# Fusing two MLP layers on one core: high and low weight halves stored side by side, column by column

## The reference

```python
w = softmax(weight, axis=-1)                       # 8 heads x 7 taps
x = causal_conv(x, w)                              # (2, 4096, 192) -> 8192 rows of 192
h = x @ moe_w_in;   x = maximum(0.01 * h, h) @ moe_w_out
h = x @ moe2_w_in
g = where(h >= 1, h, where(h <= -1, 0, (h + 1) ** 2 / 4))
out = g @ moe2_w_out                               # (8192, 192)
```

## Time and profile before

| | us |
|---|---|
| median of the runs | 1129.92 (1129.71 to 1130.29) |
| the profiled execution, its own time | 1129.76 |
| its span, from first to last instruction | 1128.0 |
| PE busy | 1116.7 (99%) |
| PEld busy | 921.9 (82%) |
| DVE busy | 896.7 (79%) |
| ACT busy | 798.2 (71%) |
| POOL busy | 50.0 (4%) |

### The profile page before, as it was taken

The page is one execution under the profiler, slowest core; times in us unless marked ns, Lnnn a source line. Parts: engine busy times, 40 slices in busy tenths (PEclk is TensorE's granted clock), DMA queues, the critical chain, the costliest instruction groups (busy, mean ns, idle before and its releaser), DMA issues.

```text
span 1128.0 us, 25723 instructions
## 1 busy us (share of the span) xinstructions
PE 1116.7 (99%) x9754; PEld 921.9 (82%) x9754; DVE 896.7 (79%) x1511; ACT 798.2 (71%) x1472; POOL 50.0 (4%) x76
## 2 busy tenths in 40 slices
PE   7999999999999999999999999999999999999998
PEld 6788888888888888888888888888888888888886
DVE  7787887888777887788877888787787877888665
ACT  6778667586675867758577685866758667686785
POOL 5543000000000000000000000000000000000000
PEclk9999999999999999999999999999999999999999
DMA  6330010101001010010100101001010100100001
GB/s 143 98 81 2 11 20 1 30 2 23 7 1 31 1 30 1 1 30 1 29 1 6 25 1 29 1 12 19 1 29 1 24 8 1 29 1 15 1 1 28
DMA packets 114568, 21.98 MB, mean 19 GB/s; under 512 B 106256, under 2 KB 114448, under 8 KB 114448
## 3 DMA queue, kind: packets, MB, share of 16 engines
q1 hardware_dynamic: 111600, 19.61, 9.7%
q10 hardware_dynamic: 2848, 0.75, 0.4%
HBM read 14.05 MB, written 6.29 MB: 18 GB/s over the span
## 4 chain that ended last, share of the span: by engine, by line
PE 96%; DVE 2%; ACT 1%; DMA 1%; issue 0%; ACTq 0%
PE acc_main L521 9%; PE acc_main L525 9%; PE acc_main L523 9%; PE acc_edge L513 9%; PE acc_edge L515 9%; PE hidden L443 9%; PE hidden L441 9%; PE hidden L445 9%; PE hidden L450 9%; PE hidden L457 5%; PE hidden L429 1%; PE acc_edge L487 1%; PE acc_main L497 1%; PE acc_main L493 1%; PE acc_main L495 1%; PE hidden L423 1%
## 5 line engine op out<-in xcount | busy, mean ns | idle before, releaser
L694 ACT CAST g_hi<-g 128x512 fp32r<-128x512 f32 x510 | 299.2, 618 | 271.9 <-PE acc_main L525 202.2
L963 DVE TENSOR_TENSOR g_lo<-g,g_hi 128x512 fp32r<-128x512 f32 x510 | 334.7, 690 | 95.8 <-ACT g_hi L694 91.2
L957 DVE SCALAR_TENSOR_TENSOR g<-hidden,pre 128x512 f32<-128x512 f32 x256 | 176.6, 690 | 105.2 <-ACT pre L682 102.3
L429 PE MATMUL hidden<-op_edge,w_edge 64*128 64x512 f32 x768 | 255.7, 386 | 0.0
L423 PE MATMUL hidden<-op_hi,w_main 64*128 64x512 f32 x512 | 198.0, 387 | 3.3 <-DVE g L952 1.8
L441 PE MATMUL hidden<-op_hi,w_main 64*128 64x512 f32 x512 | 198.2, 387 | 0.0
L445 PE MATMUL hidden<-op_hi,w_main 64*128 64x512 f32 x512 | 197.9, 386 | 0.0
L425 PE MATMUL hidden<-op_lo,w_main 64*128 64x512 f32 x512 | 197.8, 386 | 0.0
L443 PE MATMUL hidden<-op_lo,w_main 64*128 64x512 f32 x512 | 197.7, 386 | 0.0
L450 PE MATMUL hidden<-op_edge,w_edge 64*128 64x512 f32 x512 | 197.7, 386 | 0.0
L427 PE MATMUL hidden<-op_hi,w_main 64*128 64x512 f32 x512 | 197.7, 386 | 0.0
(11 more groups left out here) (128 smaller groups left out, 2775.0 us busy)
## 6 DMA issues: line engine op xcount, KB each, us to landing
x_in<-in_x_dram SPq DMA_DIRECT2D x67, 64.0 KB, 2.2
out_dram<-y_main SPq DMA_DIRECT2D x62, 64.0 KB, 1.8
stage<-in_moe_w_out_dram SPq DMA_DIRECT2D x15, 192.0 KB, 2.7
x_in_edge<-in_x_dram SPq DMA_DIRECT2D x66, 32.0 KB, 2.0
out_dram<-y_edge SPq DMA_DIRECT2D x32, 64.0 KB, 1.8
stage<-in_moe_w_in_dram SPq DMA_DIRECT2D x15, 128.0 KB, 2.4
stage<-in_moe_w_in_dram SPq DMA_DIRECT2D x30, 64.0 KB, 2.4
stage<-in_moe_w_out_dram ACTq DMA_DIRECT2D x1, 192.0 KB, 4.5
```

Of the source, the lines that this page charges most:

```text
L429: done = nc.tensor.matmul(h[:], w_edge[l][top, i - 3, cols], op_edge[l][b][top, :], start=False, stop=False)
L694: nc.scalar.copy(hi_of(n, c)[:], g[c % SLOTS][:]).then_inc(g_hi_ready, 1)
L963: nc.vector.tensor_tensor(lo_of(n, c)[:], g[c % SLOTS][:], hi_of(n, c)[:].bitcast(F32), ALU.subtract).then_inc(g_lo_ready, 1)
```

## The change

Each weight's high and low part become neighbours. `w_main` and `w_edge` become [128, 2048, 2]; `w_out` becomes [128, 8, 3, 128, 2]: for a pair of chunks a block of main columns of the first chunk, one of the second (each column high, low), and a block of edge columns in which the innermost index is the chunk of the pair, with the high parts in columns 0 to 63 and the low ones in 64 to 127. A weight load still takes 128 columns, but steps 8 bytes from one to the next, over 1024 bytes of each partition. Sizes are unchanged, and so are all buffers' addresses. The number and order of matmuls, loads, DMAs and waits stay. Elementwise instructions that write weights now write (and POOL also reads) with an 8-byte step. ACT's third instruction of a piece becomes two, one of 256 columns and one of 128; in this last one, and in POOL's fourth, the staged input is read with the chunk as innermost index.

```diff
-        w_main = [sb(f"w_main{l}", [P, 2, F], F32R) for l in (0, 1)]
-        w_edge = [sb(f"w_edge{l}", [P, 2, F], F32R) for l in (0, 1)]
-        w_out = [sb(f"w_out{l}", [P, CHUNKS, 2 * D], F32R) for l in (0, 1)]
+        w_main = [sb(f"w_main{l}", [P, F, 2], F32R) for l in (0, 1)]
+        w_edge = [sb(f"w_edge{l}", [P, F, 2], F32R) for l in (0, 1)]
+        w_out = [sb(f"w_out{l}", [P, PAIRS, 3, P, 2], F32R) for l in (0, 1)]
...
-                nc.gpsimd.tensor_tensor(main[:, 1], s[:, 0:PW], main[:, 0].bitcast(F32), ALU.subtract)
+                nc.gpsimd.tensor_tensor(main[:, :, 1], s[:, 0:PW], main[:, :, 0].bitcast(F32), ALU.subtract)
...
-                nc.gpsimd.tensor_tensor(wo[:, :, 2 * P:], rows[:, :, 0:P], wo[:, :, 0:P].bitcast(F32), ALU.subtract)
-                nc.gpsimd.tensor_tensor(wo[:, :, D:2 * P], rows[:, :, P:D], wo[:, :, P:D].bitcast(F32),
-                                        ALU.subtract).then_inc(stage_used, 1)
+                nc.gpsimd.tensor_tensor(wo[:, 0:2, :, 1], rows[:, :, 0:P], wo[:, 0:2, :, 0].bitcast(F32), ALU.subtract)
+                nc.gpsimd.tensor_tensor(wo[:, 2, EDGE:P, :], rows[:, :, P:D].rearrange("p k c -> p c k"),
+                                        wo[:, 2, 0:EDGE, :].bitcast(F32), ALU.subtract).then_inc(stage_used, 1)
...
-                    nc.tensor.matmul(h[:], w_main[l][top, 0, cols], op_hi[l][b][top, :], start=True, stop=False)
+                    nc.tensor.matmul(h[:], w_main[l][top, cols, 0], op_hi[l][b][top, :], start=True, stop=False)
...
-                    nc.tensor.matmul(edge[:], w[:, P:2 * P], hi, start=k == 0, stop=False)
+                    nc.tensor.matmul(edge[:], w[:, 2, :, k % 2], hi, start=k == 0, stop=False)
...
-                    nc.tensor.matmul(main[:], w[:, 2 * P:], hi, start=False, stop=False)
+                    nc.tensor.matmul(main[:], w[:, k % 2, :, 1], hi, start=False, stop=False)
...
-                nc.scalar.copy(main[:, 0], s[:, 0:PW]).then_inc(weights_hi, 1)
-                nc.scalar.copy(edge[:, 0], s[:, PW:2 * PW]).then_inc(weights_hi, 1)
-                nc.scalar.copy(wo[:, :, 0:D], rows).then_inc(weights_hi, 1)
+                nc.scalar.copy(main[:, :, 0], s[:, 0:PW]).then_inc(weights_hi, 1)
+                nc.scalar.copy(edge[:, :, 0], s[:, PW:2 * PW]).then_inc(weights_hi, 1)
+                nc.scalar.copy(wo[:, 0:2, :, 0], rows[:, :, 0:P])
+                nc.scalar.copy(wo[:, 2, 0:EDGE, :], rows[:, :, P:D].rearrange("p k c -> p c k")).then_inc(weights_hi, 1)
```

More of the change, by code:

```diff
@@ L246, in piece_parts @@
             cols = slice(q * PW, (q + 1) * PW)
-            return (s, w_main[l][:, :, cols], w_edge[l][:, :, cols],
-                    s[:, 2 * PW:].rearrange("p (c d) -> p c d", d=D), w_out[l][:, q * PC:(q + 1) * PC])
+            return (s, w_main[l][:, cols, :], w_edge[l][:, cols, :],
+                    s[:, 2 * PW:].rearrange("p (c d) -> p c d", d=D), w_out[l][:, q])
         same = g[3][:, 0:P]
@@ L449, in bottom_first @@
                         pe.wait_ge(op1_ready, 1)
-                    done = nc.tensor.matmul(h[:], w_edge[l][bottom, 0, cols], op_edge[l][b][bottom, :],
+                    done = nc.tensor.matmul(h[:], w_edge[l][bottom, cols, 0], op_edge[l][b][bottom, :],
                                             start=False, stop=last)
@@ L456, in bottom_first @@
                         pe.wait_ge((op1_top_ready, op2_top_ready)[l], t + 1)
-                    nc.tensor.matmul(h[:], w_edge[l][bottom, 1, cols], op_top[l][b][bottom, :],
+                    nc.tensor.matmul(h[:], w_edge[l][bottom, cols, 1], op_top[l][b][bottom, :],
                                      start=False, stop=True).then_inc(hidden_ready, 1)
@@ L483, in top_second @@
                     pe.wait_ge(g_hi_ready, CHUNKS * n + k + 1)
[L484 removed]
+                    nc.tensor.matmul(edge[:], w[:, 2, :, k % 2], hi, start=k == 0, stop=False)
                 elif i in (1, 3):
                     pe.wait_ge(g_lo_ready, CHUNKS * n + k + 1)
[L487 removed]
+                    done = nc.tensor.matmul(edge[:], w[:, 2, :, k % 2], lo, start=False, stop=False)
                     if i == 3:
@@ L507, in bottom_second @@
                 last = c == CHUNKS - 2
-                w, hi, lo = w_out[l][bottom, k], g_hi[k % SLOTS][bottom, :], g_lo[k % SLOTS][bottom, :]
+                w, hi, lo = w_out[l][bottom, k // 2], g_hi[k % SLOTS][bottom, :], g_lo[k % SLOTS][bottom, :]
                 edge, main = acc_edge[a], acc_main[a]
@@ L512, in bottom_second @@
                         pe.wait_ge(edge_top_added, PAIRS * n + c // 2 + 1)
-                    nc.tensor.matmul(edge[:], w[:, P:2 * P], hi, start=False, stop=False)
+                    nc.tensor.matmul(edge[:], w[:, 2, :, k % 2], hi, start=False, stop=False)
                 elif i in (1, 3):
-                    done = nc.tensor.matmul(edge[:], w[:, P:2 * P], lo, start=False, stop=last and i == 3)
+                    done = nc.tensor.matmul(edge[:], w[:, 2, :, k % 2], lo, start=False, stop=last and i == 3)
                     if i == 3:
@@ L520, in bottom_second @@
                         pe.wait_ge(main_top_added, PAIRS * n + c // 2 + 1)
-                    nc.tensor.matmul(main[:], w[:, 0:P], hi, start=False, stop=False)
+                    nc.tensor.matmul(main[:], w[:, k % 2, :, 0], hi, start=False, stop=False)
                 elif i in (5, 8):
-                    nc.tensor.matmul(main[:], w[:, 2 * P:], hi, start=False, stop=False)
+                    nc.tensor.matmul(main[:], w[:, k % 2, :, 1], hi, start=False, stop=False)
                 else:
-                    done = nc.tensor.matmul(main[:], w[:, 0:P], lo, start=False, stop=last and i == 9)
+                    done = nc.tensor.matmul(main[:], w[:, k % 2, :, 0], lo, start=False, stop=last and i == 9)
                     if i == 9:
@@ L542, in whole_main @@
                 last = c == CHUNKS - 1
-                w, hi, lo = w_out[l][:, c], hi_of(n, c)[:], lo_of(n, c)[:]
+                w, hi, lo = w_out[l][:, c // 2, c % 2], hi_of(n, c)[:], lo_of(n, c)[:]
                 pe.wait_ge(g_hi_ready, CHUNKS * n + c + 1)
-                nc.tensor.matmul(acc_main[a][:], w[:, 0:P], hi, start=False, stop=False)
-                nc.tensor.matmul(acc_main[a][:], w[:, 2 * P:], hi, start=False, stop=False)
+                nc.tensor.matmul(acc_main[a][:], w[:, :, 0], hi, start=False, stop=False)
+                nc.tensor.matmul(acc_main[a][:], w[:, :, 1], hi, start=False, stop=False)
                 pe.wait_ge(g_lo_ready, CHUNKS * n + c + 1)
-                done = nc.tensor.matmul(acc_main[a][:], w[:, 0:P], lo, start=False, stop=last)
+                done = nc.tensor.matmul(acc_main[a][:], w[:, :, 0], lo, start=False, stop=last)
                 if last:
```

24 lines of the change are left out of this document (12 added, 12 removed).

## The result

The changed kernel takes 1161.45 us (1161.38 to 1162.22), against 1129.87 for the kernel before beside it: a ratio of 1.028, interval 1.0263 to 1.0298. The forecast of 1130.9 did not come. The time is that of the rival "The two streams fall out of step", 1162, which had a chance of 0.08; whether its mechanism was right too is what the experiments are about. The profiled execution took 1161.38 us, 1159.6 of them span: 31.6 more than before.

The account below looks back on a forecast made before the run. PE, busy 99% of the span, was taken as the bound, at a 226.7 ns pitch. Profiled 1129.76 + 0 (pitch) + 1.0 (ACT) + 0 (steps) = 1130.8, plus 0.16 to the median, gave 1130.9; range 1118 to 1197.

Parts of the forecast that it names:

- The two streams fall out of step: Rival on PE: a longer load breaks the settled relation in time, pitch 233 ns, +31 us, 1162; chance 0.08.
- turn-taking: Rival on PE: 64 load groups cost the data stream 64 clocks instead of 32, pitch 240.0, +65 us, 1196; chance 0.15.
- The pitch: PE's step from one half-matmul pair to the next, 226.7 ns over 4864 steps, forecast unchanged: 0 us.
- Two rows speak for the latter: Argument on PE's pitch: load-free matmul records of 0.39 us and 385 ns show the 13.3 ns extra belongs to the data stream.
- the end of the 114.51 one cannot come from a successor: Defence of the load-free matmul's recorded 0.39 us at PE's stall, though ends are modelled: no successor follows it there.
- the 32 clocks: PE pitch beyond 512 columns at 2.4 GHz, 13.3 ns: either the load interrupting the stream or the stream's own.
- stays at 226.7: Forecast case for PE: load and stream independent, pitch unchanged, 0 us; chance 0.51.
- vanished clocks: Rival on PE: load and stream avoid each other's reads, pitch 216 ns, -52 us, 1079; chance 0.15.
- The load as bound: Rival on PE: the weight load outgrows its 222 ns cover; at three times its length 328 ns, +493 us, 1624; chance 0.05.
- The load's length: PE's weight load: 108 ns before, 113 forecast, bounds 108 to 216, hidden up to 222; recorded mean 184 to 189.
- ACT's split: w_out's copy on ACT becomes two: +0.12 us per piece, five on the opening chain and three in job 2, 1.0 us.
- Strided writes: Elementwise writes with a step on ACT and POOL: taken as 0; upper bound twice the time per column, ACT 3.6 us.

Follow-up runs that it names:

- the stages: Three kernels running PE alone through stages of 28 to 40 steps of one kind, computing nothing of the model; fp32r pitches with 512 data columns from 226.7 to 245 ns.
- e7_offsets: PE alone, 44 stages of 28 steps, weights displaced at 4- and 8-byte steps; 227 to 234 ns at 4 bytes, none under 230 at 8.
- e5_stages: PE alone, 32 stages of 36 matmuls with rests between, varying weight-data distances and load sizes; 4-byte loads displaced by 32 and 128 bytes 233 ns, by 256 and 512 227.

## Why the prediction was wrong

The measured time lies inside the stated range, but no term of the forecast put it there: the range's upper end came from turn-taking, which the runs exclude.

**The pitch: this is the step that failed.** It was put at 226.7 ns and 0 us, and measured 233.3 and 31.3 us. "Two rows speak for the latter" took the recorded 0.39 us of a load-free matmul as proof that a load costs the stream nothing, and from there that the layout doesn't matter. Two things were wrong in it. The record first: in the changed kernel a matmul with no load behind it stands in the timeline of PE just ahead of a stall,
```profile
116.69 0.39 PE L443 MATMUL hidden<-op_lo,w_main 64*128 64x512 f32 x1
...
117.10 0.51 PE L487 MATMUL acc_edge<-g_lo,w_out 64*128 64x512 f32 x1
```
with the same 0.39 as its neighbours that do have one. Their recorded lengths in ns, first of the prediction's own example at 114.51 in the kernel before, then of the one at 116.69 in the changed kernel:
```profile
L443 PE MATMUL hidden<-op_lo,w_main x1: 394/394/394, 114.5 to 114.5; 64*128 64x512 f32 x1
...
L443 PE MATMUL hidden<-op_lo,w_main x1: 393/393/393, 116.7 to 116.7; 64*128 64x512 f32 x1
```
Without a load they are recorded longer than the means of 386 and 392, and alike in both kernels. The L521 group moved from 386 to 392 ns when the pitch moved by 6.6. So the recorded length went with the pitch and told nothing of a load; that "the end of the 114.51 one cannot come from a successor" did not save the argument. The inference second: even if the 32 clocks are the stream's own, as the stages' equal 120.0 and 173.3 ns for both steps suggest, the *relation* of load and stream can still add to them, and it does.

**The evidence was there, and underweighted.** The earlier trace rows showed the pitch of full rows at 233 just after a stall and 226 later, and the prediction said that the settled pitch "depends on some relation in time that a longer load could break". Its price, 31 us and 1162, is what came. Its mechanism was half right: it is a relation, but one that addresses decide, and no longer load is needed to break it: the 16-byte displacement does so with a load of the same length. Time takes part, as the rival said: after a rest even a fast stage (L94 of `e7_offsets`) has, behind its first step, five of 229 to 236 ns before it settles. That the price fitted so well is in part luck: outside the fast case the runs have anything from 3 ns (the changed kernel, weights 64 bytes up) to 12 (the 16-byte step), and nothing shows why this layout costs just what a step after a stall does. Given that 1 ns was worth 4.9 us and that the earlier trace rows contained both values, 0.08 was too little and 0.51 for "stays at 226.7" too much.

**Turn-taking** (1196) and **vanished clocks** (1079) did not come. The first is excluded by 256 and 384 data columns and by the 16-byte displacement. **The load as bound** did not come either: at 212 ns (16-byte step) the load was still hidden, in keeping with the 222 worked out.

**The load's length was right**: two loads in a row, on the timeline of PEld at the stall of job 2,
```profile
117.10 0.19 PEld L487 LDWEIGHTS acc_edge<-g_lo,w_out 64*128 64x128 f32 x1 [0.45 <-DVE g_lo L964]
...
117.22 0.20 PEld L484 LDWEIGHTS acc_edge<-g_hi,w_out 64*128 64x128 f32 x1
```
are 0.12 us apart, and the group's mean is 192 where 189 was forecast. The rate of the data stream was a good guide to the load's. By the Trainium skill (SBUF — State Buffer, Specifications (TRN2)) two hits per 16-byte line keep full bandwidth. The load's 114 to 118 ns for 108 agree with that but for some 7%, and 165 and 212 ns were measured at 12 and 16 bytes, where a line has fewer hits. But the first half of the rule, read as "the time doesn't move", was wrong here. The same page of the Trainium skill (Who interferes with whom) has PE waiting for nobody, with a read port of its own for weights. The 16-byte displacement speaks against using that as a rule for the pitch, since the address of a load moved the data's pitch by 6.6 ns.

**ACT's split** cost 0.53 per piece on the chain to the next start (26.09 to 26.62) against 0.41, as forecast. Only its number of places was off: three on the chain, as the first two pieces were covered by DVE, and no sign of one in job 2. The takeover came 0.52 us later instead of 0.6 (the value of 45.71 against 46.23); of the 0.4 more in job 2 nothing shows, as the stretch behind the takeover grew by no more than its pitch explains. **Strided writes** were put at nothing; the groups by line show
```profile
L758 ACT CAST w_main<-stage 128x256 fp32r<-128x256 f32 x16 | 6.8, 426 | 1.0 <-DMA stage<-in_moe_w_out_dram 0.9
...
L386 POOL TENSOR_TENSOR w_out<-stage,w_out 128x256 fp32r<-128x256 f32 x16 | 12.0, 751 | 0.0
```
where before they had 403 and 740 ns: 6% and 1.5%. On the chain a piece takes 1.16 to 1.18 us (25.44 to 26.62 is one), where it took 1.03 before: with the split's 0.11 the step's share is about 0.03, and three pieces are 0.42 of the 0.52 at the takeover.

**Two small sums don't come out**, and neither decides anything. A gain of 2 ns of pitch gives 1130.9 - 9.7 = 1121, not 1118. And with twice the time per instruction POOL would finish piece 1's low part of w_in at about 18.9 instead of 15.02, 3 us after 15.68 and not 2.

**What stays open.** What is shown is which arrangements are fast and which aren't, not why. Of all that was measured with 512 data columns, 227 ns came only with a load of 128 neighbouring columns, at a distance from the data that is a multiple of 256 bytes; the one exception is 16 bytes below the line, fast in the stages' pairs, 228 in their full rows (L102 of `e5_stages`) and slow in the kernel. Such a distance isn't always enough: with weights and data both 16 bytes up the stages are slow and the kernel fast. A clash of the load's and the stream's reads in something that repeats every 256 bytes would fit; it was not measured, and why the changed kernel's steps alternate between 229 and 238 ns is open too. Nor was it tried whether another order of weights inside a load, or another spacing between data buffers, gives 8-byte steps the fast pitch: none of 19 different offsets did.

## What to carry to other kernels

When PE is busy 99% of the span, price a change in layout by the pitch of its matmuls, over a window of hundreds of them, and try the one address experiment (a 16-byte pad) before arguing from recorded lengths: here they followed the pitch and showed nothing of what set it. Start with each fp32 weight load on 128 neighbouring columns and at a multiple of 256 bytes from the data that it runs beside; the pads cost no time here, and being off by 16 bytes cost 2.6%. If a profile of before shows two values of the pitch for the same matmul, give a good chance to the slower one becoming the rule when the operands' layout changes, as it did here.

## What the runs showed of the hardware

- The pitch of an fp32r matmul of 512 columns depends on where its weights lie: 226.7 ns at best, 233.3 with the same weights 16 bytes off, in a kernel whose loads are otherwise well hidden (+29.9 us).
- What a matmul takes beyond its columns at 2.4 GHz isn't in proportion to them: 120.0 ns for 256 columns and 173.3 for 384 are both 13.3 more than 106.7 and 160.0, with either step.
- A weight load occupies 108, some 115, 165 and 212 ns for 128 columns in steps of 4, 8, 12 and 16 bytes, and is hidden behind a stream of 512 columns in each case, as the pitch stays at 227 to 239 ns.
- Fewer columns to load can be slower: with 64 and 32 columns a matmul took 230 and 232 ns, and with 120 columns 233, where 128 took 226.7.
- Top and bottom half streams keep their own pitch: 227 ns with 4-byte loads on top and 233 with 8-byte loads below, side by side in one stage.
